# Scan chain of a gated-state kernel on GpSimd: three instructions per step in place of four from the sixth group on, fed by turned columns from ScalarE

## The reference, cut to what matters

```python
a_n = (a_re, a_im) * min(mag, 0.999) / (mag + 1e-6)       # complex decay of each step and channel
for t in range(S):
    new_re = ar * S_re - ai * S_im                         # state S is 48 x 48, complex
    new_im = ar * S_im + ai * S_re
    S_re, S_im = (new_re + outer(k_t, v_t), new_im)
    y[t] = q_t @ S_re
```

## Time and profile before

| what | value |
|---|---|
| median of three runs | 907.92 us |
| the profiled execution itself | 906.64 us |
| its span in the trace | 904.9 us |
| granted TensorE clock, mean | 0.96 of 2.4 GHz |
| PE / DVE / POOL / ACT busy, share of the span | 88% / 71% / 56% / 53% |
| busy tenths of POOL in 40 slices (22.6 us each) | 1199989799999999999985000003323333234322 |
| busy tenths of DVE in the same slices | 5989789899797989899887755277332353547821 |

### The profile page before, as it was taken

The page is one execution under the profiler, slowest core; times in us unless marked ns, Lnnn a source line. Parts: engine busy times, 40 slices in busy tenths (PEclk is TensorE's granted clock), DMA queues, the critical chain, the costliest instruction groups (busy, mean ns, idle before and its releaser), DMA issues.

```text
span 904.9 us, 18765 instructions
## 1 busy us (share of the span) xinstructions
PE 798.0 (88%) x6641; PEld 740.6 (82%) x6642; DVE 641.8 (71%) x1046; ACT 483.0 (53%) x977; POOL 508.3 (56%) x873
## 2 busy tenths in 40 slices
PE   0567898988988999999999999949999999999995
PEld 0435887878878888888899999938999999997894
DVE  5989789899797989899887755277332353547821
ACT  5685857776766767776545654234211242436611
POOL 1199989799999999999985000003323333234322
PEclk9769899999999999999999999977999999999998
DMA  9401152453424242423311110445511142417211
GB/s 305 130 11 43 32 146 76 117 132 96 116 76 110 77 111 93 112 76 84 86 51 56 56 41 22 159 150 184 192 35 49 50 153 79 154 59 269 97 36 45
DMA packets 41876, 89.74 MB, mean 99 GB/s; under 512 B 6264, under 2 KB 23680, under 8 KB 40480
## 3 DMA queue, kind: packets, MB, share of 16 engines
q1 hardware_dynamic: 37632, 76.04, 27.7%
q0 software_dynamic: 4160, 12.60, 4.2%
HBM read 69.74 MB, written 17.69 MB: 97 GB/s over the span
## 4 chain that ended last, share of the span: by engine, by line
PE 51%; POOL 17%; DVE 17%; issue 7%; ACT 4%; DMA 2%; ACTq 0%; DVEq 0%; SPq 0%; POOLq 0%
POOL c_im L2102 5%; POOL c_re L2101 4%; PE yu L1731 4%; PE yu L1735 4%; PE yu L1732 4%; POOL ring L2105 4%; PE mm L1731 4%; POOL ring L2104 4%; PE mm L1735 3%; PE mm L1732 3%; PE tr L2003 2%; PE mm L2004 2%; PE tr L2004 2%; PE mm L2003 2%; PE mm L2005 2%
## 5 line engine op out<-in xcount | busy, mean ns | idle before, releaser
L1731 PE MATMUL mm<-up_hi,x_hi 128*128 128x384 f32 x432 | 156.4, 362 | 3.0 <-DVE h_sb L1194 2.6
L1732 PE MATMUL mm<-up_lo,x_hi 128*128 128x384 f32 x432 | 147.5, 341 | 0.0
L2101 POOL TENSOR_TENSOR c_re<-ring 112x128 f32<-112x128 f32 x165 | 106.0, 642 | 58.0 <-DVE ring L1147 36.4
L2178 POOL DMA_INDIRECT out_rows<-g_o,rows_out x30 | 35.3, 1176 | 145.4 <-DVE g_o L1583 132.4
L2102 POOL TENSOR_TENSOR c_im<-ring 112x128 f32<-112x128 f32 x165 | 114.4, 693 | 0.0
L1735 PE MATMUL mm<-up_hi,x_lo 128*128 128x384 f32 x432 | 99.8, 339 | 1.2 <-DVE x_lo L1182 1.2
L2105 POOL TENSOR_TENSOR ring<-c_re,c_im 112x64 f32<-112x64 f32 x165 | 97.0, 588 | 0.0
L2104 POOL TENSOR_TENSOR ring<-c_re,c_im 112x64 f32<-112x64 f32 x165 | 88.0, 533 | 12.9
L2154 POOL DMA_INDIRECT g_in<-x_scratch,rows_in x34 | 37.9, 1114 | 94.1 <-DVE rows_in L1546 69.0
L1731 PEld LDWEIGHTS mm<-up_hi,x_hi 128*128 128x128 f32 x432 | 82.5, 191 | 8.2 <-issue 4.3
L1194 DVE TENSOR_TENSOR h_sb<-mm,h_sb 128x384 f32<-128x384 f32 x96 | 52.8, 550 | 44.0 <-PE mm L1735 43.8
(11 more groups left out here) (261 smaller groups left out, 2242.7 us busy)
## 6 DMA issues: line engine op xcount, KB each, us to landing
raw<-in_moe_w SPq DMA_DIRECT2D x16, 1536.0 KB, 9.1
a_dn<-in_a_laid SPq DMA_DIRECT2D x18, 384.0 KB, 7.1
an_scratch<-a_dn SPq DMA_DIRECT2D x18, 384.0 KB, 2.3
ring<-an_scratch SPq DMA_DIRECT2D x18, 384.0 KB, 5.6
q_in<-in_q_laid SPq DMA_DIRECT2D x24, 224.0 KB, 2.8
k_in<-in_k_laid SPq DMA_DIRECT2D x24, 224.0 KB, 3.1
v_in<-in_v_laid SPq DMA_DIRECT2D x24, 192.0 KB, 3.2
x_scratch<-x_sb SPq DMA_DIRECT2D x24, 192.0 KB, 2.0
```

What stands on the lines that cost most here:

```text
L1731: nc.tensor.matmul(out, hi[:, x, :], w_hi(x), start=(x == 0), stop=False)
L1732: nc.tensor.matmul(out, hi[:, x, :], w_lo(x), start=False, stop=False)
L2101: nc.gpsimd.tensor_tensor(c_re[:, 0:count, :, :], cur, bc(prev[:, :, 0, :], 2, 2), ALU.mult).then_inc(chain_prod, 1)
```

## The change

A group from `TURNED` = 5 on (the sixth, counted from 0; seven groups, 105 steps) is chained in three instructions a step. ACT writes, ahead of POOL, a copy `turn` of the columns with the planes crossed and the sign in it: plane 0 is minus the imaginary part, plane 1 the real part. POOL then forms column times real part (128 elements), turned column times imaginary part (128) and one addition of 128 elements over both planes. `turn` holds eight columns of each of the four blocks, so ACT writes it in quarters of four columns (the first has three), two activations each: quarter 0 at the end of ACT's iteration 2g-5, quarter 1 ahead of `y_copy` in 2g-4, quarter 2 at the end of 2g-4, quarter 3 ahead of `y_copy` in 2g-3. Quarter 0 waits for the ring's load; each waits until POOL has used the quarter that it overwrites. POOL waits for a quarter at steps 1, 4, 8 and 12. `turns(g-1)` moves from after step 12 to after step 11 for these groups. The semaphore of the steps counts one per step instead of two (`links_after`). To make room, three small tiles become parts of others (the router's embedding lies in `st_x`, the fallback's selectors in `n_sq`), and the two product tiles shrink to the four blocks used.

```diff
@@ tiles
-        c_re = sb1("c_re", [R, 8, 2, W])
-        c_im = sb1("c_im", [R, 8, 2, W])
+        c_re = sb1("c_re", [R, NBLK, 2, W])
+        c_im = sb1("c_im", [R, NBLK, 2, W])
+        turn = sb1("turn", [R, NBLK, 2 * QUARTER, 2, W])
...
+        def links_after(done):
+
+            return 2 * done - max(0, done - steps_before(TURNED))
...
@@ ScalarE
+            def turn_quarter(g, part):
+
+                if not TURNED <= g < NG:
+                    return
+                if part == 0:
+                    act.wait_ge(pads_loaded, 16 * min(RING, max(RING - DIRECT, g + 1 - DIRECT)))
+                    act.wait_ge(ring_loaded[g % RING], 32 * (g // RING + (1 if g % RING >= DIRECT else 0)))
+                old, at = g - (1 if part < 2 else 0), (part + 2) % 4
+                if old >= TURNED:
+                    act.wait_ge(chain_prod, 2 * (steps_before(old) + (at + 1) * QUARTER - 1))
+                first = max(1, part * QUARTER)
+                count, to = (part + 1) * QUARTER - first, first % (2 * QUARTER)
+                for x in range(2):
+                    nc.scalar.activation(turn[:, :, to:to + count, x, :], ring_b[:, g % RING, :, first:first + count, 1 - x, :], ACT.Copy,
+                                         scale=1.0 if x else -1.0).then_inc(turn_ready, 1)
@@ ScalarE's loop
                 if n == 0:
                     low_copy(range(14, 16))
+                if now and n % 2 == 0:
+                    turn_quarter(n // 2 + 2, 1)
+                if now and n % 2 == 1:
+                    turn_quarter((n + 3) // 2, 3)
                 if now and n >= 1:
                     y_copy(n)
...
                 if more and n >= 5:
                     rotation(n + 1)
+                if now and n % 2 == 0:
+                    turn_quarter(n // 2 + 2, 2)
+                if now and n % 2 == 1:
+                    turn_quarter((n + 5) // 2, 0)
                 for m in norms if not maxima_first(n) else ():
                     norm_rest(m, norm_of(m))
@@ VectorE, join
-                    dve.wait_ge(chain_step, 2 * (steps_before(g) + steps_of(g)))
+                    dve.wait_ge(chain_step, links_after(steps_before(g) + steps_of(g)))
@@ GpSimd, chain_steps
-                    wait(pool, chain_step, 2 * done)
+                    wait(pool, chain_step, links_after(done))
                     nc.gpsimd.tensor_tensor(c_re[:, 0:count, :, :], cur, bc(prev[:, :, 0, :], 2, 2), ALU.mult).then_inc(chain_prod, 1)
+                    if g >= TURNED:
+                        if j == 1 or j % QUARTER == 0:
+                            pool.wait_ge(turn_ready, 2 * (4 * (g - TURNED) + j // QUARTER + 1))
+                        nc.gpsimd.tensor_tensor(c_im[:, :, :, :], turn[:, :, j % (2 * QUARTER), :, :], bc(prev[:, :, 1, :], 2, 2), ALU.mult).then_inc(chain_prod, 1)
+                        pool.wait_ge(chain_prod, 2 * (done + 1))
+                        nc.gpsimd.tensor_tensor(cur, c_re[:, :, :, :], c_im[:, :, :, :], ALU.add).then_inc(chain_step, 1)
+                        continue
...
             for g in range(3, NG):
-                chain_steps(g, range(1, 13))
+                most = 13 if g < TURNED else 12
+                chain_steps(g, range(1, most))
                 turns(g - 1)
-                chain_steps(g, range(13, BLK))
+                chain_steps(g, range(most, BLK))
```

More of the change, by code:

```diff
@@ L22 @@
 NBLK = HALF // BLK
+QUARTER = BLK // 4
+TURNED = 5
 DIRECT = 3
@@ L86, in attention_moe_program @@
         low = sb("low", [1, 1], I32)
-        sel_v = sb("sel_v", [P, D])
-        sel_y = sb("sel_y", [D, P])
         sel_all = sb("sel_all", [D, 3 * P])
-        emb_sb = sb("emb_sb", [E, HD])
         emb_s = sb("emb_s", [E, 8])
@@ L151, in attention_moe_program @@
         emb_sq = x2_sb[0:E, :]
+        emb_sb = st_x[0:E, :, :, :].rearrange("e x h d -> e (x h d)")
+        spare = n_sq[:, :, :, :].rearrange("p i x w -> p (i x w)")
+        sel_v, sel_y = spare[:, 0:D], spare[0:D, P:2 * P]
         phase1.close()
@@ L246, in attention_moe_program @@
         chain_step = sem("chain_step")
+        turn_ready = sem("turn_ready")
         span_prod = sem("span_prod")
```

## The result

The changed kernel takes 911.67 us (median of 7 runs, 910.54 to 913.0) against 908.85 us for the kernel before in the same sessions (907.36 to 910.57). The ratio is 1.0031, 95% interval 1.0019 to 1.0043: 2.8 us slower, where 3.65 us faster had been forecast. The kernel before took 0.9 us more here than the 907.92 us that the forecast started from. The measured time lies above the forecast's range of 899.5 to 910.5 us, and by 0.2 us it still would with the range moved up by 0.9.

A forecast was written before the change was run, and what follows sets the result against it. Bound taken: POOL's chain to 290 us with DVE nearly as late, a DVE-ACT-PE ring to 450, then PE. Terms -0.75 - 1.6 + 1.5 - 2.8 = -3.65 us from 907.92 gave 904.3 us, range 899.5 to 910.5.

The forecast's parts named there:

- Part 1: POOL's chain: a step falls from 2,528 ns to about 2.1 us, giving POOL 8.5 us of rest per group.
- Part 2: ACT's turned copies: 0.42 us each, 0.75 a quarter, hidden in iterations 9 to 16, costing nothing there.
- Part 3: Four steps behind quarter 3: 0.5 us of new wait at joins 7, 8 and 9, +1.5 us.
- Part 4: Old waits shrink: -1.6 us at join(6, 0) in iteration 9, -0.75 us in iteration 7.
- Part 5: DVE's two-SBUF-input instructions relieved by POOL's rest: 0.7 us per pair, four pairs in iterations 10 to 17, -2.8 us.
- Rival (b): Longer POOL instructions eat DVE's relief, leaving 0.2 of 0.7 us a pair: no change, 906.3 us; chance 0.23.
- rival (a): Last quarter becomes the bound at join(g, 0): +4.2 us, 912; chance 0.20 together with POOL not being shortened.

The follow-up runs named there:

- copies_only: Kernel before, chain in four instructions, plus ACT's turned copies made from a constant tile and read by nobody: 907.38 us against 909.32, ratio 0.9983.
- after_split: Changed kernel, quarters in their places, its addition of 128 elements split into two of 64: 913.95 us against 908.28 for the kernel before, ratio 1.0066.
- meet: Separate test, DVE products beside GpSimd products or memsets: with two SBUF inputs 0.60 us alone, 0.73, 0.86 and 1.13 beside 64, 128 and 256 elements.
- layout_only: Kernel before with the change's tiles alone, no copies, chain as before: 908.35 us against 909.02, ratio 0.9990.
- early_split: The early kernel with its addition of 128 elements split into two of 64: 907.82 us against 909.02 for the kernel before, ratio 0.9988.
- early kernel: Changed kernel with three of the four quarters written half an iteration sooner: 911.62 us against 909.32 for the kernel before, ratio 1.0024.

## Why the prediction was wrong

- **Part 1 (POOL's step) held.** 2.1 us forecast, 2.16 measured; the addition 0.655 and 0.69; rest per group 8.5 us forecast, 7 to 8 measured. The rest fits in part by luck: the forecast took the new group by the sum of its instructions (32.8 us) from the old one with its gaps (41.3); 15 steps shorter by 0.43 are 6.4 us, and the rest is longer because a group now takes some 43 us.
- **Part 2 (ACT's copies) held.** 0.40 us each, 0.71 a quarter (0.42 and 0.75 forecast), no wait for POOL or the ring, and copies_only shows them free.
- **Part 3 (the last quarter) held, on the good side.** Four steps end where DVE arrives; no wait instead of 0.5 us. But that is luck: the last step ends 16.0 us after iteration 11 begins (318.66), 0.3 later than forecast, and DVE is there so late because its own late part has grown; in the kernel before it was there after 15.55. The two may hang together: GpSimd's last product takes 1.45 us (332.71) beside DVE's k_t (332.46), for 0.46 alone. after_split shows what the mechanism costs when a step is longer.
- **Part 4 (the old waits) held for the waits and not for the time.** 2.14 us at join 6 and most of 2.36 us at x_lo went (0.36 stayed). Late part 9 fell by 1.44 us (12.13 to 10.69) and iteration 7 by 0.52. But iterations 6 and 8 grew, 8 by 0.77 us, and early part 9 by 0.77; from iteration 5 to 10 the two traces take 111.4 and 111.9 us (111.6 in the second profile of the kernel before, where iteration 6 takes 25.12 us: 1.0 of the 1.7 us that it grew is the execution's). The forecast had priced waits only, not the longer instructions around them.
- **Part 5 (DVE's relief) is the step that failed.** It took the time in which POOL rests as the only difference (-2.8 us), and said of it that it falls "where DVE waits for nobody". Two errors: in the early part of even iterations DVE would wait for PE as soon as it is sooner (0.80 us in iteration 14), so that relief is worth nothing; and in the late parts, where it would be worth something, POOL works all the time and each meeting costs 0.12 to 0.14 us more. In the traces that is +3.2 us in late parts and +0.2 in early ones from iteration 10 to 16, instead of -2.8. The part's count of 32 instructions was low too: beside joins, z and decays it has 6, but x_lo, st_t and four of the norm's are 12 in two iterations.
- **Rival (b)** had the right mechanism and a wrong size. Half of an instruction's length, 0.23 for 0.20 us, was too mild. By meet a meeting costs 0.26 us with 128 elements and 0.12 with 64, so with the old mixture of two and two, weighted by their time, about 0.20 (an estimate): 0.06 more, not 0.03. k_in and k_t grew by 0.14 and 0.12, more than that. It also left 0.2 us of relief a pair where there is none. With the 3.2 us of the late parts and no new wait at the joins its sum is -0.75 - 1.6 + 3.2 = +0.85 us, on the other side.
- The forecast's bound for part 5, "from below nothing", was what kept the range's upper side tied to rival (a) alone. The row that spoke against it was there: DVE's l_re at 0.824 for 0.683 us is a cost per meeting, and it had to be asked what a meeting with the *other* instruction costs, and in which part of the iteration.

**What stays open.** The two profiles differ by 4.9 us at the last answers and the medians by 2.8 us; the profiled execution of before was 2.2 us below its median of 908.85, that of the change near its own, and which part of an execution varies so wasn't followed further. Why copies_only is 1.5 us faster than before isn't settled either. In its trace the gain stands between iterations 5 and 10, with GpSimd's chain for group 6 sooner against DVE; layout_only takes 111.5 us there and has the wait of 2.15 us, so the tiles alone don't do it. What makes the chain sooner isn't shown. Whether the turned columns alone (c_im read from another tile) shorten the late part to 9.90 us in early_split wasn't tried apart.

## What to carry to other kernels

Where two engines exclude each other on memory reads, fewer and longer instructions on the side engine can cost the one on the path more than many short ones: count meetings times the cost of one, not busy time. Split the path engine's iteration at the point where another engine holds it: relief ahead of that point turns into a wait, though work moved there can still cost (in the early kernel 11.75 us for 11.06). Before a copy is made a condition for a chain, measure how much of the chain still fits between the copy and its reader.

## What the runs showed of the hardware that was not expected

A DVE product of 512 elements with two SBUF inputs came every 0.60 us alone and every 0.73, 0.86 and 1.13 us beside GpSimd products of 64, 128 and 256 elements: in turns, at GpSimd's own time plus 0.45 us. For short instructions the cost of a meeting so grows faster than their length (0.12 to 0.26 us, where GpSimd's own time goes from 0.28 to 0.41). Beside memsets of 512 elements, which read nothing, and with one input in PSUM, it stayed at 0.60 us.

Beside a dense run of GpSimd products of 256 and then 512 elements one DVE instruction stood for 37.3 us and was passed over by 32 of them: what it waits for isn't always one instruction of the other engine.
